# The gated stage's spatial mix as seven half-size products (one level of Strassen) in place of eight

## The chip, the cores and the metric

One Trainium2 chip, one core of it. The time is device microseconds of one execution; the number compared is the median over runs. A profiled execution gives the trace.

## The reference, cut to what matters

```python
# stage 1: a recurrence over 768 positions of 4 batches x 8 heads, state 40 x 40 (a chunked form in the kernel)
x = attention(r, k, v, w, a, b)                    # (4, 768, 320)
# stage 2: the gated block
h = np.maximum(x @ w_in, 0.0)                      # (4, 768, 1024)
u, v = h[..., :512], h[..., 512:]
v_n = (v - mean(v)) / np.sqrt(var(v) + 1e-06)      # over the 512 features of a row
v_s = np.einsum('ts,bsd->btd', w_spatial, v_n) + b_spatial[None, :, None]   # the spatial mix, 768 x 768
y = (u * v_s) @ w_out                              # (4, 768, 320)
# stage 3: a router picks one of 8 experts for each row (a row may keep its predecessor's expert),
# out = p[e] * (np.maximum(y @ w1[e], 0) @ w2[e])
```

All of it is float32.

## The kernel before, in words

The kernel is one program in which each engine has its own hand-written order of work, with semaphores between them. Stage 1 goes through 24 chunks of 32 positions and ends near 352 us. Stage 2 follows batch by batch, stage 3 tile by tile (31 tiles of 128 rows sorted by expert).

For one batch of stage 2 TensorE first makes `values` (v, six tiles of 128 tokens, 512 columns, relu'd by ScalarE into `self.v`), then the output rows `outs` of the batch before, then `gates` (u, transposed: features on partitions, 384 tokens per block, relu'd by ScalarE into `self.g`), then the spatial mix. In between VectorE has the norm of v (`norm`, in place) and, for the batch before, `routing.choose`.

The mix (`mix`, L226) works on transposed blocks: `self.v[:, s, d*128:...]` is the stationary operand, `self.wspT[:, s, t*384:...]` the moving one, s runs over the six tiles of tokens, and block j = (d, t) has d = j % 4 (128 features) and t = j // 4 (half of the 768 tokens). It fills one of two PSUM banks (D) in turns; `wait_ge(self.vs_out, n - 1)` holds a block until the gate has read the bank's last content. For each block VectorE's `gate` adds the bias out of PSUM (L293) and multiplies the gate's block in `self.g` by the sum (L297), which raises `gated`. `outs` needs all four blocks of its half of the tokens.

The routing of the batch before is spread over the mix. TensorE turns rows for it after gates j = 4 (`turn_rows`), turns the chosen experts back after mix j = 2 (`turn_back`), and counts after mix j = 3 (`count`). VectorE has, in its one queue, gate 0, `scan`, gates 1 and 2, `weigh`, gates 3 and 4, `place` (and in the last batch `first_tiles`, the table of the first eleven expert tiles), and gates 5 to 7. `scan` runs over 768 positions on one partition; SyncE's `split_rows` and `join_rows` carry its input and its result by small DMAs, and TensorE's `turn_back` waits for the latter. `weigh` waits for the turned experts, `count` for `weigh`'s one-hot rows, `place` for the counts. GpSimd scatters the batch's rows once `place` is through; SyncE fetches the first expert tiles when the scatters have landed and `first_tiles` is through.

After the last batch's mix TensorE goes on with its six output groups (L238), with the first two x tiles of stage 3 turned behind groups 3 and 4, and then with the first expert tile. `woutT` and `wgl` lie in `w1_own` during stage 1; TensorE multiplies them (`fold`) at its end and ScalarE copies the result (L157, raising `fold_d`).

Of the kernel before, what the change touches and what calls it, by code (L numbers as in the profile page):

```python
# [8 lines left out]
F32 = mybir.dt.float32  # L9
I32 = mybir.dt.int32  # L10
U32 = mybir.dt.uint32
ALU = mybir.AluOpType
# [3 lines left out]
P = 128  # L16
# [8 lines left out]
E_FF = 1024  # L25
# [21 lines left out]
GROUPS2 = TILES + 2 * ND  # L47
REST = KCH[-1][1]
# [25 lines left out]
class Gated:  # L74
# [4 lines left out]
    def __init__(self, nc, ctx, room, rows, banks, x_rows, w_in, w_spatial, b_spatial, w_out, w_gate, w_local):  # L79
# [6 lines left out]
        self.v, self.vs, self.bsp = low("v", TILES, D_HALF), low("vs", 2, TH), low("bsp", SEQ)  # L86
# [5 lines left out]
        self.wout, self.g, self.rows = sb("wout", ND, ROW), sb("g", ND, SEQ), rows  # L92
        self.stats, self.mv = sb("stats", TILES, 6), sb("mv", TILES, 2)
        self.sd, self.rs, self.half_sd, self.var = (sb(n, TILES) for n in ("sd", "rs", "half_sd", "var"))
        A, B, D, G, E = banks
        self.pair_banks = {"GE": (G[:, :], E.rearrange("p a i t -> p (a i t)")), "B": (B[:, 0], B[:, 1]),
                           "D": (D[:, 0], D[:, 1])}
        self.vs_bank, self.o_bank = (D[:, 0], D[:, 1]), (B[:, 0], B[:, 1])
# [6 lines left out]
        self.stat, self.rooted, self.normed, self.gated = sem("stat"), sem("rooted"), sem("normed"), sem("gated")  # L105
# [110 lines left out]

    def mix(self, pe, b, j):
        d, t, n = j % ND, j // ND, 2 * ND * b + j
# [4 lines left out]
        if n >= 2:  # L223
            pe.wait_ge(self.vs_out, n - 1)
        for s in range(TILES):
            mm = pe.matmul(self.vs_bank[n % 2][:, 0:TH], self.v[:, s, d * P:(d + 1) * P],  # L226
                           self.wspT[:, s, t * TH:(t + 1) * TH], start=(s == 0), stop=(s == TILES - 1))
        mm.then_inc(self.vs_made, 1)

    def outs(self, pe, b, i):  # L230
        n = TILES * b + i
        pe.wait_ge(self.gated, 2 * ND * b + ND * (1 + i * P // TH))
# [55 lines left out]
    def gate(self, dve, b, j):  # L288
        d, t, n = j % ND, j // ND, 2 * ND * b + j
        cols = slice(t * TH, (t + 1) * TH)  # L290
        dve.wait_ge(self.biased, 16)
        dve.wait_ge(self.vs_made, n + 1)
        dve.tensor_tensor(self.vs[:, n % 2, :], self.vs_bank[n % 2][:, 0:TH], self.bsp[:, cols],  # L293
                          ALU.add).then_inc(self.vs_out, 1)
        dve.wait_ge(self.vs_out, n + 1)
        dve.wait_ge(self.h_out, self.u_at(b, j) + 1)
        dve.tensor_tensor(self.g[:, d, cols], self.g[:, d, cols], self.vs[:, n % 2, :],  # L297
                          ALU.mult).then_inc(self.gated, 1)
# [376 lines left out]
def all_stages(nc, room, banks, inputs, x_rows, gated, side, routing, experts_w, experts):  # L675
# [3 lines left out]
    with ExitStack() as ctx:  # L679
# [83 lines left out]
        with nc.Block() as block:  # L763
# [79 lines left out]
            def _(pool):  # L843
# [78 lines left out]
                routing.constants(pool)  # L922
# [778 lines left out]
```

## Time and profile before

| | |
|---|---|
| median of 3 runs | 962.45 us (962.36 to 962.65) |
| the profiled execution, its own time | 962.87 us |
| its span, first to last instruction | 961.20 us |
| mean granted TensorE clock | 0.988 |
| busy: TensorE, VectorE, ScalarE, GpSimd | 935.0, 434.2, 250.9, 243.9 us |

A span is the time between the first and the last instruction. PE is TensorE (matmuls), PEld its weight loads, DVE VectorE, ACT ScalarE, POOL GpSimd, SP SyncE; a q behind an engine's name is its queue of DMAs. L226 is line 226 of the kernel. A float32 matmul stands as two records. In brackets behind a row of a timeline stands the idle time ahead of it and what ended it.

### The profile page before, as it was taken

How to read it: one execution, taken by the hardware profiler on the slowest of the kernel's cores; microseconds unless marked ns; L12 is line 12 of the kernel's file. 1: busy time of each engine (PE TensorE's matmuls, PEld its weight loads, DVE VectorE, ACT ScalarE, POOL GpSimd, SP SyncE). 2: the span in 40 equal slices, each digit the busy share in tenths (PEclk: the TensorE clock that was granted, in tenths of full speed). 3: DMA queues.
4: the chain of work that ended last, by engine and by line, in shares of the span. 5: the costliest groups of instructions: out<-in, count | busy, mean ns of one | idle time of the engine just before them, and what ended most of it. 6: DMA issues, size and time to landing. Idle time of an engine off the chain costs nothing.

```text
span 961.2 us, 54005 instructions
## 1 busy us (share of the span) xinstructions
PE 935.0 (97%) x24701; PEld 722.6 (75%) x24702; DVE 434.2 (45%) x958; ACT 250.9 (26%) x527; POOL 243.9 (25%) x226
## 2 busy tenths in 40 slices
PE   6999999999999999999999999999999999999995
PEld 6888999999999984545545555558878888888884
DVE  5476777777777633332333333253343222222220
ACT  0234444444444432002102102102122121212120
POOL 6444555445545410000020020020251011111101
PEclk8999999999999999999999999999999999999998
DMA  4265554544443325910110110329131110101000
GB/s 114 78 201 153 153 158 117 156 137 129 124 129 117 101 53 151 324 50 1 50 41 1 49 42 1 100 88 320 49 104 36 35 40 29 30 22 41 23 28 3
DMA packets 61396, 86.00 MB, mean 89 GB/s; under 512 B 22706, under 2 KB 40958, under 8 KB 61344
## 3 DMA queue, kind: packets, MB, share of 16 engines
q1 hardware_dynamic: 37232, 63.30, 21.6%
q10 hardware_dynamic: 21088, 13.32, 5.2%
q0 software_dynamic: 3024, 8.72, 2.5%
q8 instruction: 28, 0.46, 0.2%
q14 instruction: 24, 0.20, 0.1%
HBM read 72.47 MB, written 14.45 MB: 90 GB/s over the span
## 4 chain that ended last, share of the span: by engine, by line
PE 96%; issue 2%; DVE 1%; POOL 0%; ACT 0%; DVEq 0%; POOLq 0%; ACTq 0%
PE ps_D L1495 14%; PE ps_D L226 12%; PE ps_G L1477 6%; PE ps_E L1477 6%; PE ps_B L238 6%; PE ps_E L983 5%; PE ps_B L190 3%; PE ps_G L1484 3%; PE ps_D L1018 3%; PE ps_D L955 3%; PE ps_E L981 3%; PE ps_G L190 3%; PE ps_E L190 2%; PE ps_D L1056 2%; PE ps_B L960 2%; PE ps_A L960 2%
## 5 line engine op out<-in xcount | busy, mean ns | idle before, releaser
L1495 PE MATMUL ps_D<-room,hT 128*128 x496 | 139.1, 433 | 0.8 <-issue 0.8
L226 PE MATMUL ps_D<-room 128*128 128x384 f32 x384 | 126.7, 489 | 0.7 <-DVE room L293 0.7
L1495 PEld LDWEIGHTS ps_D<-room,hT 128*128 128x128 f32 x496 | 91.8, 190 | 35.9 <-issue 1.3
L226 PEld LDWEIGHTS ps_D<-room 128*128 128x128 f32 x384 | 72.1, 190 | 51.5 <-issue 1.6
L1438 POOL DMA_INDIRECT out<-y,token x31 | 35.6, 1147 | 258.3 <-DVE y L1602 225.0
L552 POOL DMA_INDIRECT sorted_rows<-rows,slot x24 | 23.9, 997 | 280.4 <-DVE slot L544 274.3
L1538 ACT ACTIVATE hT<-ps_G 128x512 f32<-128x512 f32 x31 | 18.6, 599 | 217.3 <-PE ps_E L1484 211.1
L1602 DVE TENSOR_SCALAR y<-ps_D,x_in 128x320 f32<-128x320 f32 x31 | 17.0, 550 | 126.6 <-PE ps_D L1495 118.1
L1585 DVE COPY w_own<-room 128x1024 f32 x62 | 44.8, 727 | 62.8 <-PE ps_G L1477 32.7
L293 DVE TENSOR_TENSOR room<-ps_D,room 128x384 f32<-128x384 f32 x32 | 17.8, 558 | 113.2 <-PE ps_D L226 108.2
L1237 DVE STREAM_TRANSPOSE room<-room 128x256 f32<-128x256 f32 x96 | 42.3, 441 | 53.5 <-ACT room L1125 53.5
L1477 PEld LDWEIGHTS ps_G<-xTt,w_own 128*128 128x128 f32 x496 | 59.9, 192 | 6.5 <-issue 2.3
L1477 PE MATMUL ps_G<-xTt,w_own 128*128 128x128 f32 x496 | 60.7, 276 | 1.5 <-issue 0.9
L1477 PE MATMUL ps_E<-xTt,w_own 128*128 128x128 f32 x496 | 60.5, 275 | 0.0
L1477 PEld LDWEIGHTS ps_E<-xTt,w_own 128*128 128x128 f32 x496 | 57.9, 192 | 0.0
L238 PE MATMUL ps_B<-room 128*128 128x329 f32 x192 | 54.6, 441 | 0.0
L909 POOL TENSOR_TENSOR room<-room 128x640 f32<-128x640 f32 x23 | 46.4, 2019 | 29.6 <-DVE room L1285 29.6
L885 POOL TENSOR_TENSOR room<-room 128x1024 f32<-128x1024 f32 x24 | 52.2, 2174 | 1.9
L1125 ACT ACTIVATE room<-ps_E 128x256 f32<-128x256 f32 (+1 forms) x96 | 35.0, 365 | 66.0 <-PE ps_E L983 37.3
L238 PEld LDWEIGHTS ps_B<-room 128*128 128x128 f32 x192 | 36.0, 190 | 18.4 <-issue 2.3
L983 PE MATMUL ps_E<-room 32*32 32x48 f32 (+1 forms) x3200 | 48.5, 207 | 0.8 <-issue 0.8
L1125 ACT ACTIVATE room<-room 128x512 f32<-128x512 f32 (+2 forms) x72 | 40.3, 560 | 34.5 <-PE ps_B L1034 31.1
(224 smaller groups left out, 1599.3 us busy)
## 6 DMA issues: line engine op xcount, KB each, us to landing
room<-in_moe_w SPq DMA_DIRECT2D x8, 1280.0 KB, 13.3
room<-in_moe_w SPq DMA_DIRECT2D x8, 1024.0 KB, 10.1
room<-in_vt SPq DMA_DIRECT2D x24, 320.0 KB, 3.2
room<-in_kb SPq DMA_DIRECT2D x46, 160.0 KB
x_in<-sorted_rows ACTq DMA_DIRECT2D x27, 161.0 KB, 2.2
room<-in_vo SPq DMA_DIRECT2D x24, 160.0 KB, 3.0
room<-in_rg SPq DMA_DIRECT2D x48, 80.0 KB
room<-in_r SPq DMA_DIRECT2D x48, 80.0 KB
```

What stands on the lines that cost most here:

```text
L190: pe.matmul(self.bank_of(n + g)[:, 0:width], left(g, k, slice(0, P)), right(g, k, slice(0, P)), start=(k == 0), stop=False, skip_group_che ...
L226: mm = pe.matmul(self.vs_bank[n % 2][:, 0:TH], self.v[:, s, d * P:(d + 1) * P], self.wspT[:, s, t * TH:(t + 1) * TH], start=(s == 0), stop ...
L238: mm = pe.matmul(self.o_bank[n % 2][:, 0:ROW], self.g[:, d, i * P:(i + 1) * P], self.wout[:, d, :], start=(d == 0), stop=(d == ND - 1))
L885: pool.tensor_tensor(kb_end.rearrange("p m n k t -> p (m n) k t"), raw_kb[:, :, :, :], later[:, :, None, :].broadcast_to([P, GROUPS, 2, CH ...
L909: pool.tensor_tensor(faded.rearrange("p m n e -> p (m n) e")[:, :, 0:HD], stateT.rearrange("p m n e -> p (m n) e"), whole[:, x % 4, :, Non ...
L960: mm = pe.transpose(bank[0:kept, m // 4, m % 4 * P:m % 4 * P + LIVE], src(m), ident[0:LIVE, 0:LIVE])
L983: mm = pe.matmul(E[q, :, i, kept], pw[q, i, :], powers[q, l - 2:ROUNDS - 1:ROUNDS - l, i, kept], start=True, stop=True)
L1125: act.activation(out, in_, ACT.Copy).then_inc(done, 1)
L1237: dve.transpose(pw.rearrange("p i t -> p (i t)"), (powers[:, l - 1] if l else qi[:, 0]).rearrange("p i t -> p (i t)")).then_inc(flip_d[l], 1)
L1477: mm = pe.matmul(self.ps_h[half][:, f, :], side.w1_own[:, k, col:col + P], x[:, k, :], start=(f == 0 and k == 0), stop=False, skip_group_c ...
L1495: mm = pe.matmul(self.ps_y, side.hT[:, u % 2, f, :], self.weights.w2[:, bass.ds(e, 1), f, :], start=(f == 0), stop=(f == self.NF - 1))
L1585: dve.tensor_copy(side.w1_own[:, :, cols], w1.w1[:, bass.ds(e, 1), :, cols].rearrange("p o k f -> p (o k) f")).then_inc(self.w1_in, 1)
```

## The change

The mix is a product of the 512 x 768 matrix v (transposed) and the 768 x 768 matrix of weights. Both are cut in quarters (`parts`): w into halves of the tokens summed over and of the tokens produced, v into halves of tokens and of features. Strassen's seven products of quarters replace the eight. Each product has three token tiles in place of six to sum over; each is made in two pieces c of 128 features, so a batch has 14 (`PRODUCTS`) of them, each with three matmuls of 128x128 by 384.

- Weights: five sums of quarters on GpSimd, once, four behind its constants (`sum_weights`), one when the fold is copied (`sum_last_weights`), since it lies in `w1_own`.
- Values: five sums of quarters on VectorE in each batch behind the norm (`sum_values`), ahead of `choose`.
- `gate`: each product is added to or subtracted from up to two partial sums of 384 columns in SBUF (`lower_left`, `upper_right`, `first`, `second`); four of seven products in each piece complete a block, which `times` multiplies into `self.g`. `gated` becomes a pair of semaphores, one for each half of the tokens.
- A third PSUM bank, A[:, 1], joins the two of D. TensorE's wait for `fold_d` moves ahead of the first mix; in the last batch the wait for all banks moves to the output group 3.
- The routing's steps move: `scan` behind gate 1, `weigh` behind gate 5, `place` and `first_tiles` behind gate 10; `turn_back` behind product 4, `count` behind product 8.
- New buffers lie in `hT`, in `w1_own` and in a new tensor `sums`; the scratch for software DMA is cut to 4096 bytes a partition.

```diff
+ST = TILES // 2
+PRODUCTS = 14
...
+        self.w_parts, self.v_parts = self.parts(self.wspT, TH), self.parts(self.v, D_HALF // 2)
+        sb = Carver(side.hT.rearrange("p a f n -> p (a f n)"), 0, 2 * E_FF)
+        w_top, more = sb("w_top", ST, TH), sb("more", 2, TH)
+        self.upper_right, self.lower_left, self.first, self.second = vs[:, 0], vs[:, 1], more[:, 0], more[:, 1]
+        sb = Carver(ctx.enter_context(nc.sbuf_tensor("sums", [P, ST * (TH + D_HALF)], F32)), 0, ST * (TH + D_HALF))
+        w_bottom, v_late, v_early = sb("w_bottom", ST, TH), sb("v_late", ST, D_HALF // 2), sb("v_early", ST, D_HALF // 2)
+        sb = Carver(side.w1_own.rearrange("p k f -> p (k f)"), 0, (NK - 1) * E_FF)
+        w_both, v_both = sb("w_both", ST, TH), sb("v_both", ST, D_HALF // 2)
+        self.w_sums, self.v_sums = (w_top, w_bottom, w_both), (v_early, v_late, v_both)
...
-        self.vs_bank, self.o_bank = (D[:, 0], D[:, 1]), (B[:, 0], B[:, 1])
+        self.vs_bank, self.o_bank = (D[:, 0], D[:, 1], A[:, 1]), (B[:, 0], B[:, 1])
...
+    def parts(self, x, width):
+
+        return [[x[:, i * ST:(i + 1) * ST, j * width:(j + 1) * width] for j in range(2)] for i in range(2)]
...
+    def sum_weights(self, pool):
+        (w11, w12), (w21, w22) = self.w_parts
+        top, bottom, both = self.w_sums
+        pool.wait_ge(self.loaded, 16 * self.transfers)
+        pool.tensor_tensor(top, w11, w12, ALU.add).then_inc(self.w_summed, 1)
+        pool.tensor_tensor(bottom, w21, w22, ALU.add).then_inc(self.w_summed, 1)
+        pool.wait_ge(self.w_summed, 2)
+        pool.tensor_tensor(w21, w21, w11, ALU.subtract).then_inc(self.w_summed, 1)
+        pool.tensor_tensor(w12, w12, w22, ALU.subtract).then_inc(self.w_summed, 1)
+
+    def sum_last_weights(self, pool, fold_d):
+        (w11, w12), (w21, w22) = self.w_parts
+        pool.wait_ge(fold_d, 1)
+        pool.tensor_tensor(self.w_sums[2], w11, w22, ALU.add).then_inc(self.w_summed, 1)
+
+    def sum_values(self, dve, b):
+
+        (v11, v21), (v12, v22) = self.v_parts
+        early, late, both = self.v_sums
+        dve.wait_ge(self.normed, TILES * (b + 1))
+        for k, (out, x, y, op) in enumerate(((early, v11, v12, ALU.add), (late, v21, v22, ALU.add),
+                                             (both, v11, v22, ALU.add), (v12, v12, v22, ALU.subtract),
+                                             (v21, v21, v11, ALU.subtract))):
+            if k == 3:
+                dve.wait_ge(self.v_summed, 5 * b + 3)
+            dve.tensor_tensor(out, x, y, op).then_inc(self.v_summed, 1)
+
+    def product(self, j):
+
+        (v11, v21), (v12, v22) = self.v_parts
+        (w11, w12), (w21, w22) = self.w_parts
+        (w_top, w_bottom, w_both), (v_early, v_late, v_both) = self.w_sums, self.v_sums
+        return ((v22, w21, 4, 0), (v11, w12, 4, 0), (v_early, w22, 4, 1), (v_late, w11, 4, 2), (v_both, w_both, 5, 3),
+                (v12, w_bottom, 5, 4), (v21, w_top, 5, 5))[j % 7]
+
     def mix(self, pe, b, j):
-        d, t, n = j % ND, j // ND, 2 * ND * b + j
+        n, c = PRODUCTS * b + j, j // 7
+        left, right, weights, values = self.product(j)
         if j == 0:
             pe.wait_ge(self.normed, TILES * (b + 1))
             if b == 0:
                 pe.wait_ge(self.h_out, self.u_at(0, ND) + 2)
-        if n >= 2:
-            pe.wait_ge(self.vs_out, n - 1)
-        for s in range(TILES):
-            mm = pe.matmul(self.vs_bank[n % 2][:, 0:TH], self.v[:, s, d * P:(d + 1) * P],
-                           self.wspT[:, s, t * TH:(t + 1) * TH], start=(s == 0), stop=(s == TILES - 1))
+        if b == 0 and c == 0:
+            pe.wait_ge(self.w_summed, weights)
+        if values and c == 0:
+            pe.wait_ge(self.v_summed, 5 * b + values)
+        if n >= 3:
+            pe.wait_ge(self.vs_out, n - 2)
+        for s in range(ST):
+            mm = pe.matmul(self.vs_bank[n % 3][:, 0:TH], left[:, s, c * P:(c + 1) * P], right[:, s, :],
+                           start=(s == 0), stop=(s == ST - 1))
         mm.then_inc(self.vs_made, 1)
...
     def outs(self, pe, b, i):
-        pe.wait_ge(self.gated, 2 * ND * b + ND * (1 + i * P // TH))
+        pe.wait_ge(self.gated[i * P // TH], ND * (b + 1))
...
     def gate(self, dve, b, j):
-        d, t, n = j % ND, j // ND, 2 * ND * b + j
-        cols = slice(t * TH, (t + 1) * TH)
-        dve.wait_ge(self.biased, 16)
+
+        n, c, which = PRODUCTS * b + j, j // 7, j % 7
+        made = self.vs_bank[n % 3][:, 0:TH]
+        ur, ll, one, two = self.upper_right, self.lower_left, self.first, self.second
+        if n == 0:
+            dve.wait_ge(self.biased, 16)
         dve.wait_ge(self.vs_made, n + 1)
-        dve.tensor_tensor(self.vs[:, n % 2, :], self.vs_bank[n % 2][:, 0:TH], self.bsp[:, cols],
-                          ALU.add).then_inc(self.vs_out, 1)
+        if n >= 1:
+            dve.wait_ge(self.vs_out, n)
+
+        def plus(out, x, op=ALU.add):
+            return dve.tensor_tensor(out, x, made, op)
+
+        if which == 0:
+            plus(ll, self.bsp[:, 0:TH]).then_inc(self.vs_out, 1)
+        elif which == 1:
+            plus(ur, self.bsp[:, TH:]).then_inc(self.vs_out, 1)
+        elif which == 2:
+            plus(two, ur)
+            plus(one, ll, ALU.subtract).then_inc(self.vs_out, 1)
+            self.times(dve, b, n, c, 1, two)
+        elif which == 3:
+            plus(ll, ll)
+            plus(ur, ur, ALU.subtract).then_inc(self.vs_out, 1)
+            self.times(dve, b, n, 2 + c, 0, ll)
+        elif which == 4:
+            plus(one, one)
+            plus(ur, ur).then_inc(self.vs_out, 1)
+        elif which == 5:
+            plus(one, one).then_inc(self.vs_out, 1)
+            self.times(dve, b, n, c, 0, one)
+        else:
+            plus(ur, ur).then_inc(self.vs_out, 1)
+            self.times(dve, b, n, 2 + c, 1, ur)
+
+    def times(self, dve, b, n, d, t, factor):
+        g = self.g[:, d, t * TH:(t + 1) * TH]
         dve.wait_ge(self.vs_out, n + 1)
-        dve.wait_ge(self.h_out, self.u_at(b, j) + 1)
-        dve.tensor_tensor(self.g[:, d, cols], self.g[:, d, cols], self.vs[:, n % 2, :],
-                          ALU.mult).then_inc(self.gated, 1)
+        dve.wait_ge(self.h_out, self.u_at(b, d + ND * t) + 1)
+        dve.tensor_tensor(g, g, factor, ALU.mult).then_inc(self.gated[t], 1)
...
                 routing.constants(pool)
+                gated.sum_weights(pool)
+                gated.sum_last_weights(pool, fold_d)
...
                 gated.gates(pe, 0, ND + 2)
-                for j in range(2 * ND):
+                pe.wait_ge(fold_d, 1)
+                for j in range(PRODUCTS):
                     gated.mix(pe, 0, j)
-                pe.wait_ge(fold_d, 1)
                 for b in range(1, BATCH):
                     for i in range(0, TILES, 2):
                         gated.values(pe, b, i)
...
                         gated.gates(pe, b, j)
                         if j == 4:
                             routing.turn_rows(pe, b - 1)
-                    for j in range(2 * ND):
+                    for j in range(PRODUCTS):
                         gated.mix(pe, b, j)
-                        if j == 2:
+                        if j == 4:
                             routing.turn_back(pe, b - 1)
-                        if j == 3:
+                        if j == 8:
                             routing.count(pe, b - 1)
                 experts.tensor(pe)
 
...
                 routing.convert(dve)
                 for b in range(BATCH):
                     gated.norm(dve, b)
+                    gated.sum_values(dve, b)
                     if b >= 1:
                         routing.choose(dve, b - 1)
-                    for j in range(2 * ND):
+                    for j in range(PRODUCTS):
                         gated.gate(dve, b, j)
                         if b >= 1:
-                            if j == 0:
+                            if j == 1:
                                 routing.scan(dve, b - 1)
-                            if j == 2:
+                            if j == 5:
                                 routing.weigh(dve, b - 1)
-                            if j == 4:
+                            if j == 10:
                                 routing.place(dve, b - 1)
                                 if b == BATCH - 1:
                                     routing.first_tiles(dve)
...
-        sp.wait_ge(gated.gated, 2 * ND * BATCH)
+        for done in gated.gated:
+            sp.wait_ge(done, ND * BATCH)
...
         for i in range(TILES):
             gated.outs(pe, self.LAST, i)
+            if i == 3:
+                pe.wait_ge(gated.vs_out, PRODUCTS * BATCH)
             if i >= 3 and i < 5:
                 self.turn_x(pe, 0, i - 3)
         pe.wait_ge(gated.h_out, GROUPS2 * BATCH)
-        pe.wait_ge(gated.vs_out, 2 * ND * BATCH)
...
-    nc = bacc.Bacc("TRN2", target_bir_lowering=False, num_devices=1)
+    nc = bacc.Bacc("TRN2", target_bir_lowering=False, num_devices=1, dynamic_dma_scratch_size=4096)
```

## Rows read from the trace of the kernel before

**Rows 1.** The page's busy time by engine: us, share of the span, instructions.

```profile
PE 935.0 (97%) x24701; PEld 722.6 (75%) x24702; DVE 434.2 (45%) x958; ACT 250.9 (26%) x527; POOL 243.9 (25%) x226
```

**Rows 2.** The page's chain that ended last, shares by engine.

```profile
PE 96%; issue 2%; DVE 1%; POOL 0%; ACT 0%; DVEq 0%; POOLq 0%; ACTq 0%
```

**Rows 3.** The page's groups, the mix: busy us, mean ns | idle before, releaser.

```profile
L226 PE MATMUL ps_D<-room 128*128 128x384 f32 x384 | 126.7, 489 | 0.7 <-DVE room L293 0.7
```

**Rows 4.** Timeline of VectorE in batch 0: start us, us, instruction [idle before].

```profile
404.19 0.56 DVE L293 TENSOR_TENSOR room<-ps_D,room 128x384 f32<-128x384 f32 x1 [2.72 <-PE ps_D L226]
```

**Rows 5.** Timeline of TensorE where batches 0 and 1 begin and end their mix.

```profile
388.33 4.14 PE L226 MATMUL ps_D<-room 128*128 128x384 f32 x12
...
419.40 1.88 PE L190 MATMUL ps_G<-room 128*128 128x512 f32 x4
...
461.19 11.88 PE L226 MATMUL ps_D<-room 128*128 128x384 f32 x36
...
493.05 1.88 PE L190 MATMUL ps_G<-room 128*128 128x512 f32 x4
```

**Rows 6.** Timeline of TensorE in batch 3: the mix, then the output groups.

```profile
608.49 11.88 PE L226 MATMUL ps_D<-room 128*128 128x384 f32 x36
...
641.28 9.04 PE L238 MATMUL ps_B<-room 128*128 128x329 f32 x32
```

**Rows 7.** Timeline of GpSimd's last constant and of ScalarE's copy of the fold.

```profile
343.74 0.29 POOL L417 TENSOR_SCALAR_AFFINE_SELECT upper<-upper 128x128 f32<-128x128 f32 x1
...
370.26 0.21 ACT L157 ACTIVATE room<-ps_A 128x36 f32<-128x36 f32 x1
```

**Rows 8.** GpSimd's sums at L909: duration ns min/median/max.

```profile
L909 POOL TENSOR_TENSOR room<-room x23: 1262/2091/2093, 46.5 to 341.2; 128x640 f32<-128x640 f32 x23
```

**Rows 9.** Timeline of VectorE: end of batch 0's norm, and batch 1's first routing step.

```profile
385.10 2.83 DVE L285 TENSOR_SCALAR room<-room 128x512 f32<-128x512 f32 x6
...
447.47 0.20 DVE L447 TENSOR_REDUCE top<-rows 128x6 f32<-128x48 f32 x1 [4.89 <-ACT rows L259]
```

**Rows 10.** Timeline of VectorE in batch 3: gate 0, scan, place to first_tiles, gate 5.

```profile
612.73 0.56 DVE L293 TENSOR_TENSOR room<-ps_D,room 128x384 f32<-128x384 f32 x1 [16.11 <-PE ps_D L226]
613.33 0.56 DVE L297 TENSOR_TENSOR room<-room 128x384 f32<-128x384 f32 x1
613.80 1.74 DVE L482 TENSOR_TENSOR_SCAN wide<-wide 1x768 f32<-1x768 f32 x1
...
630.08 0.25 DVE L534 TENSOR_TENSOR_SCAN upto<-inner,counts 128x48 f32<-128x48 f32 x1
...
636.70 0.56 DVE L293 TENSOR_TENSOR room<-ps_D,room 128x384 f32<-128x384 f32 x1
```

**Rows 11.** Timeline of SyncE's queue: join_rows in batch 1, the first fetches.

```profile
468.27 0.74 SPq L488 DMA_DIRECT2D turned<-wide  x1
...
642.73 3.71 SPq L1416 DMA_DIRECT2D x_in<-sorted_rows  x4
```

**Rows 12.** Busy time in one stretch; the last two columns are DMA share and GB/s.

```profile
469.60:469.90 0.30, 0.30 (x2) 0.19 (x1) 0.27 (x2) 0.00 (x0) 0.00 (x0) 1.00 0.05 10
```

**Rows 13.** DMA issues, 641 to 646 us: KB each, median us to landing.

```profile
x_in<-sorted_rows SPq DMA_DIRECT2D x3, 161.0 KB, 3.2
```

**Rows 14.** Timeline in stage 3: split_rows of the last batch and the scan behind it.

```profile
661.45 1.56 ACTq L476 DMA_DIRECT2D wide<-turned  x2
...
667.88 1.75 DVE L482 TENSOR_TENSOR_SCAN wide<-wide 1x768 f32<-1x768 f32 x1 [7.21 <-DMA wide<-turned]
```

**Rows 15.** Timeline of TensorE in stage 1, two rows behind an idle stretch.

```profile
10.72 0.35 PE L1005 MATMUL ps_A<-room 64*40 64x40 f32 x3 [2.78 <-issue]
...
73.37 0.81 PE L1028 MATMUL ps_B<-room 64*40 64x32 f32 x64 [2.90 <-issue]
```

**Rows 16.** Busy time in two stretches; third column from the end is the granted clock.

```profile
10.72:16.72 6.00, 6.00 (x181) 5.50 (x183) 2.20 (x2) 0.00 (x0) 4.64 (x6) 0.50 0.12 34
...
74.80:77.80 3.00, 3.00 (x63) 2.67 (x64) 2.05 (x3) 0.98 (x1) 2.20 (x2) 0.50 0.71 203
```

More of the change, by code:

```diff
@@ L77, with __init__ @@
     EPS = 1e-6
-    def __init__(self, nc, ctx, room, rows, banks, x_rows, w_in, w_spatial, b_spatial, w_out, w_gate, w_local):
+    def __init__(self, nc, ctx, room, side, banks, x_rows, w_in, w_spatial, b_spatial, w_out, w_gate, w_local):
         def sem(name):
@@ L85, in __init__ @@
         low = Carver(room, EARLY * EXPERT_FLOATS, FIRST_END)
-        self.v, self.vs, self.bsp = low("v", TILES, D_HALF), low("vs", 2, TH), low("bsp", SEQ)
+        self.v, vs, self.bsp = low("v", TILES, D_HALF), low("vs", 2, TH), low("bsp", SEQ)
         sb = Carver(room, FIRST_END, (EXPERTS - 1) * EXPERT_FLOATS)
@@ L91, in __init__ @@
         sb = Carver(room, (EXPERTS - 1) * EXPERT_FLOATS, ROOM)
-        self.wout, self.g, self.rows = sb("wout", ND, ROW), sb("g", ND, SEQ), rows
+        self.wout, self.g, self.rows = sb("wout", ND, ROW), sb("g", ND, SEQ), side.rows
         self.stats, self.mv = sb("stats", TILES, 6), sb("mv", TILES, 2)
         self.sd, self.rs, self.half_sd, self.var = (sb(n, TILES) for n in ("sd", "rs", "half_sd", "var"))
+        self.w_parts, self.v_parts = self.parts(self.wspT, TH), self.parts(self.v, D_HALF // 2)
[7 more added lines that the diff above has]
+        self.w_sums, self.v_sums = (w_top, w_bottom, w_both), (v_early, v_late, v_both)
         A, B, D, G, E = banks
@@ L104, in __init__ @@
         self.o_made, self.o_out = sem("o_made"), sem("o_out")
-        self.stat, self.rooted, self.normed, self.gated = sem("stat"), sem("rooted"), sem("normed"), sem("gated")
+        self.stat, self.rooted, self.normed = sem("stat"), sem("rooted"), sem("normed")
+        self.w_summed, self.v_summed, self.gated = sem("w_summed"), sem("v_summed"), (sem("gated0"), sem("gated1"))
+    def parts(self, x, width):
+        return [[x[:, i * ST:(i + 1) * ST, j * width:(j + 1) * width] for j in range(2)] for i in range(2)]
     def load(self, eng, part):
@@ L1635, in program @@
                   ctx.enter_context(nc.psum_tensor("ps_E", [P, 2, 8, CH], F32))]
-        gated = Gated(nc, ctx, room, side.rows, banks, x_rows, moe_w_in, moe_w_spatial, moe_b_spatial,
+        gated = Gated(nc, ctx, room, side, banks, x_rows, moe_w_in, moe_w_spatial, moe_b_spatial,
                       (moe_w_out, moe_w_outT), moe2_w_gate, moe2_w_local)
```

## The prediction

> **What bounds the kernel now.** I read the page's engine line first [rows 1]: TensorE is busy for 97% of the span, no other engine for half of it. The chain of waits agrees [rows 2]: 96% of what ended last is TensorE. Then the costliest groups [rows 3]: the mix keeps TensorE busy for 126.7 us and makes it wait for VectorE once, 0.7 us; VectorE's gate waits 2.72 us for TensorE ahead of each block in the undisturbed stretch [rows 4]. So time taken from the mix comes off the kernel one for one, as long as VectorE, which makes the factors, stays ahead. The question is where it falls behind.
>
> The timelines give the stage. A block of 128x384 is 12 recorded matmuls (six, two records each). From the first record to the next line's first the stage lasts 419.40 - 388.33 = 31.07 us in batch 0, 493.05 - 461.19 = 31.86 us in batch 1, whose rows batch 2 repeats [rows 5], and 641.28 - 608.49 = 32.79 us in batch 3 [rows 6]. A block takes 3.87 us: VectorE's idle of 2.72, its first instruction to the second's start (0.59) and the second's 0.56 [rows 4, 10]. Eight blocks are 30.96, 0.11 is left in batch 0. Batches 1 and 2 have 0.79 us more, TensorE's turn and count for the routing; batch 3 has 0.93 more than these, its wait for VectorE.
>
> **What is removed.** Eight blocks of 12 records become fourteen products of 6 of the same shape, 3.87/2 = 1.935 us each, 27.09 together. Each batch's stage loses 3.87 us, four lose 15.48. The group borders rise from 8 to 14; the 0.11 us left over in batch 0 bounds what eight cost, so six more cost 0 to 0.08 us. I take 0.
>
> **Weight sums on GpSimd.** Four sums of 3 x 384 = 1152 columns when its constants end at 344.03, a fifth once ScalarE has copied the fold at 370.47 [rows 7]. The nearest row is its 128x640 sum: 1.26 us at best, 2.09 in the median [rows 8], so 1152 columns cost 2.3 to 3.8 us. Four end between 353 and 359, the fifth at 374.3 at the latest, 14 us before the mix: cost 0. What they do to VectorE while the last chunk ends is bounded by 0 and the 0.83 us between those two durations; I take 0. The Trainium skill's GPSIMD Engine Reference (Specifications) speaks against such a split: GpSimd shares its SBUF interfaces with VectorE and contends with its instructions that have two SBUF inputs. By that rule the sum would be up to 0.8 us later; the spread in the row fits it and does not show the cause.
>
> **Value sums on VectorE.** Five of 768 columns after the norm. The row of 384 is 0.56 us [rows 4], so 768 cost between 0.56 and 1.12; as 384 columns more can't cost a second start, I take 0.95, 4.75 us a batch (2.8 to 5.6). The Trainium skill's page "VectorE: DVE Perf Modes" (the section on SBUF-src operations) gives a float32 tensor_tensor of N columns (N+151)/0.96 ns, 0.957 us here; by it the five are 4.8 us.
> From batch 1 on VectorE stood idle for 4.89 us after the norm, until the output rows were copied at 447.47 [rows 9]; the sums fill just that, 14 us before the mix at 461.19. Cost 0; if they take 5.6, routing's choose begins 0.7 later and TensorE turns its result 10 us later still. In batch 0 the norm ends at 387.93 [rows 9], so the sums run until 392.7 beside the mix. Products 0 and 1 need none; product 2 wants the first at 388.33 + 3.87 = 392.2, which is there at 388.9. But gate 0 queues behind all five: its bank is read out at 393.3, and product 3, the first to reuse a bank, wants that at 394.1. Cover 0.8 us, just gone at 5.6 for the five. Cost 0.
>
> **The gate's work.** Per batch it was 16 instructions of 384 columns, now 28 (20 that read a bank, 8 products). One that waits for its forerunner starts 0.59 us behind it (0.60 in the first pair), one that doesn't 0.47 to 0.48 [rows 10]. The heaviest (which = 2 and 3) take 0.48 + 0.59 + 0.48 = 1.55 us against TensorE's 1.935, and three banks leave two products of slack. In itself the gate keeps up.
>
> **The routing between gates.** The scan stood behind gate 0, whose block was seen by VectorE 612.73 - 608.49 = 4.24 us after the start (3.87 + 0.37). It now stands behind gate 1, whose product ends at the same 3.87: it starts at 4.72, lasts 1.74, ends at 6.46. SyncE's small transfer carries it back, and TensorE turns it behind product 4, at 9.68, where it was behind block 2, at 11.6. The transfer was issued at 468.27 and its bytes had moved by 469.90 [rows 11, 12]; with 0.4 for its semaphore I take 2.0, so 8.5, 1.2 us early. Gate 2, behind the scan, has read its bank by 7.6; product 5 wants it at 9.68. Weigh, eight short instructions of 0.24 us (below), is behind gate 5, whose product is seen at 12.3; gate 6 is out at 15.9, wanted at 18. Cost 0 for each.
>
> Place and first_tiles are the long block: 28 short instructions from 630.08 to 636.70, 6.62 us [rows 10]. They stood behind gate 4 of 8, with blocks 5 and 6 (7.74 us) for TensorE to work on; they now stand behind gate 10 of 14. Place alone ends batches 1 and 2, and there TensorE goes on to the next batch's values: free. In batch 3 it is not. Product 10 ends 11 x 1.935 + 0.79 = 22.08 after the start; gate 10 begins at 22.45 and its three instructions let place begin at 24.0. The block ends at 30.6. Queued behind it are gates 11 (0.48 + 0.59) and 12 (0.59 + 0.56), and the first output group waits for gate 12's factor: 32.85, on TensorE 32.9. TensorE has run out of products at 27.09 + 0.11 + 0.79 = 28.0. It stands idle for 4.9 us, and batch 3's stage is 32.9 us where it was 32.8: all of this batch's saving is given back and 0.1 more. Gate 13 ends 1.2 us later, its output group comes 6.8 us later: free.
>
> What hangs on place (scatter, then the fetch of x tiles) moves from 21.6 to 24.0 after the start, 2.4 later. The fetch went out at 642.73 [rows 11], 34.2 from the start, now 36.6; with 3.2 us to land [rows 13] it is there at 39.8. TensorE turns the first tile behind four output groups, 32.9 + 9.0 = 41.9 [rows 6]. Cover 2.1 us, cost 0. The scratch for software DMA is cut as well; no row shows what it does. What it could slow is GpSimd, busy for 25% of the span [rows 1]; I take 0, and a scatter later than the 2.1 us of cover would be paid.
>
> **The clock.** Near a TensorE that stood still the granted clock fell to 0.50, the 1.2 GHz level: from 10.72, after 2.78 us of idling, it was 0.50 for 6.0 us of work; after 2.90 us of idling up to 73.37 it was 0.50 from 74.80 to 77.80 [rows 15, 16]. The idle of 4.9 us is longer than both. Work at 1.2 GHz takes twice as long, so 3 to 6 us of it cost 1.5 to 3.0; I take 2.3. If the clock does not fall it is 0.
>
> **Sum.** 3 x 3.87 = 11.6 saved in batches 0 to 2, less 0.1 in batch 3, less 2.3 of clock: 9.2. The profiled execution takes 962.87 us (span 961.20 and 1.67 around it), so 953.7 after. The median of the runs is 0.42 lower: 953.3.
>
> **Rivals.**
> - *The stall without the clock.* TensorE waits 4.9 us but stays at 2.4 GHz. For: its 0.7 us wait in batch 3 changed nothing. Against: both waits near 3 us lowered it. 962.45 - 11.5 = 951.0.
> - *The way back is late.* The margin between scan and turn falls from 5.1 to 3.2 us, three times. For: in the last batch ScalarE had issued two such transfers by 663.01 and VectorE got them at 667.88, 4.9 us [rows 14]. Against: expert weights were loading then. At 4.9 us each turn comes 1.7 late, up to 5.1 in all: 954 to 958.4.
> - *Full saving.* VectorE's block fits after all: 962.45 - 15.5 = 947.0. It would have to begin 4.9 us earlier; nothing speaks for it.
> - *VectorE becomes the bound (slower).* Per batch 28 gate instructions and 5.5 us of scan, weigh and place stand in a stage that was 31.1 us. It decides from (31.1 - 5.5)/28 = 0.91 us each; at 1.12 (twice 0.56) a batch takes 36.9 us, 5.8 x 4 = 23 more: 985. Against: the rows of 384 columns, with an input in PSUM or both in SBUF, are all 0.56.
> - *No change.* Half-length groups cost 0.65 us more each at their six new borders. Against: 0.11 left for eight.
>
> **How the numbers follow.** My forecast 0.60 (own range 952.3 to 954.9); stall without clock 0.14; way back late 0.15; full saving 0.03; slower 0.05; no change 0.03. The range 950.5 to 957.5 takes in the first two and most of the third. 0.2% (1.9 us) is about what a measurement of this kernel can tell from no change. Faster 0.92, same 0.03, slower 0.05.
>
> **What would show it.** The mix's group at 126.7 x 7/8 = 111 us and 336 records; stages of 27.2 us in batch 0, 28.0 in 1 and 2; in batch 3 one idle of about 4.9 us before the first output group, released by VectorE's gate; the granted clock at 0.50 for some us behind it. I am wrong if TensorE waits between the products or at the turn in batches 1 and 2, if the short VectorE block is not what the output group waits for, or if the clock stays up.

## The result, and the profile after

| | before | changed |
|---|---|---|
| median | 962.44 us (962.36 to 962.65, 4 runs) | 950.57 us (949.40 to 952.38, 4 runs) |
| profiled execution, span | 962.87, 961.20 us | 952.38, 950.6 us |
| ratio | | 0.9876, 95% interval 0.9864 to 0.9889 |

The kernel is 11.9 us faster; 953.3 was forecast, with 950.5 to 957.5 as the range. The median lies at the range's very edge, outside my own narrower range of 952.3 to 954.9, and nearer to the 951.0 of the rival "the stall without the clock" than to my figure. The time alone would have picked that rival; the trace rules it out, since the clock did fall. Stage 2 came out as forecast, wait and low clock included; 1.2 to 3.3 us more came from an edit that I had priced at nothing, the cut of the DMA scratch.

The timeline of TensorE shows batch 0 from its first product to its last and the line behind it, then the ends of batch 1; these answer to [rows 5].

```profile
391.11 4.14 PE L282 MATMUL ps_D<-room 128*128 128x384 f32 x12
395.08 2.10 PE L282 MATMUL ps_A<-room,sums 128*128 128x384 f32 x6
397.02 2.10 PE L282 MATMUL ps_D<-room,sums 128*128 128x384 f32 x6
...
416.37 2.10 PE L282 MATMUL ps_D<-hT,room 128*128 128x384 f32 x6
418.30 1.88 PE L206 MATMUL ps_G<-room 128*128 128x512 f32 x4
...
460.09 2.20 PE L282 MATMUL ps_A<-room 128*128 128x384 f32 x6
...
488.08 1.88 PE L206 MATMUL ps_G<-room 128*128 128x512 f32 x4
```

Products start 1.93 to 1.94 us apart behind the first (2.04), in three banks in turns, without an idle mark. Batch 0 lasts 418.30 - 391.11 = 27.19 us, batch 1 27.99 (forecast 27.2 and 28.0); batch 2, from 529.87 to 557.86, 27.99 too.

Batch 3 answers to [rows 6]. Same view, TensorE:

```profile
599.65 4.14 PE L282 MATMUL ps_D<-room 128*128 128x384 f32 x12
...
625.71 2.10 PE L282 MATMUL ps_D<-hT,room 128*128 128x384 f32 x6
632.46 11.57 PE L294 MATMUL ps_B<-room 128*128 128x329 f32 x32 [4.66 <-DVE room L384]
643.87 0.49 PE L1553 MATMUL ps_A<-ident,x_in 128*128 128x128 f32 x3
```

And VectorE there (L620 opens place, L684 first_tiles, L356 and L384 are the gate's sum and product); it answers to [rows 10]:

```profile
623.57 0.25 DVE L620 TENSOR_TENSOR_SCAN upto<-inner,counts 128x48 f32<-128x48 f32 x1
...
625.41 0.07 DVE L684 MEMSET first<- 128x9 f32 x1
...
630.06 0.17 DVE L678 CAST tile_expert<-wide 128x11 int32<-128x11 f32 x1
630.14 0.55 DVE L356 TENSOR_TENSOR hT<-hT,ps_A 128x384 f32<-128x384 f32 x1
630.61 0.55 DVE L356 TENSOR_TENSOR room<-room,ps_A 128x384 f32<-128x384 f32 x1
631.26 0.55 DVE L356 TENSOR_TENSOR hT<-hT,ps_D 128x384 f32<-128x384 f32 x1
631.85 0.56 DVE L384 TENSOR_TENSOR room<-room,hT 128x384 f32<-128x384 f32 x1
```

Place begins 23.92 us behind the stage's start (forecast 24.0), the four gate instructions stand in a row behind first_tiles, and the last of them ends at 632.41, 0.05 ahead of the output groups. The stage lasts 32.81 us; before it was 32.79. The wait is where and as long as forecast. Behind it the 32 records of four output groups take 11.57 us where they took 9.04 [rows 6]. The busy times with the granted clock (third column from the end) say why:

```profile
632.46:636.80 4.34, 4.34 (x8) 2.85 (x9) 2.60 (x5) 0.00 (x0) 0.96 (x1) 0.50 0.20 76
640.00:645.00 5.00, 5.00 (x21) 3.49 (x20) 0.00 (x0) 1.44 (x5) 0.00 (x0) 1.00 0.94 303
```

TensorE works at 1.2 GHz at first (0.50), at 2.4 GHz again later (1.00).

The spans differ by 961.2 - 950.6 = 10.6 us. By sections: the start of the first mix comes 2.78 us later (391.11 against 388.33); from there to the output groups of batch 3 it is 11.60 us less (241.35 against 252.95); from there to the first expert tile's second product 2.53 more (clock); the tiles 1.2 less (all but 0.1 of it at tile 5, which e6 and e11 come back to); behind the last tile's second product (939.89, before 947.39) 3.1 less. The first of these can't be put down to the change: over the 13 profiles of this study, most of them with the same stage 1, the first mix starts between 387.4 and 391.1 us (both ends are kernels with the change, the two without it start at 388.3 and 389.4), and the stretches at 1.2 GHz in the first 90 us differ from one execution to the next.

The last of them is a term that the forecast did not have. GpSimd's last DMA, before, changed, and in the experiment e1:

```profile
953.43 0.98 POOL L1438 DMA_INDIRECT out<-y,token  x1 [4.40 <-DVE y L1602]
```

```profile
945.93 0.98 POOL L1528 DMA_INDIRECT out<-y,token  x1 [4.39 <-DVE y L1693]
```

```profile
955.33 0.98 POOL L1438 DMA_INDIRECT out<-y,token  x1 [4.39 <-DVE y L1602]
```

The span ends 7.8 us behind its issue before (961.2), 4.7 in the changed kernel (950.6) and 4.7 in e1 (960.0).

### The profile page after: what moved, and what is told of

It reads as the page before. It is cut to its first block, busy times and chain, and to the rows that moved or that the text cites. A ratio compares the mean times of both kernels' runs of the same rounds, so it can differ in the third digit from the quotient of the medians.

```text
span 950.6 us, 54027 instructions
## 1 busy us (share of the span) xinstructions
PE 924.5 (97%) x24653; PEld 717.5 (75%) x24654; DVE 475.2 (50%) x1026; ACT 249.8 (26%) x527; POOL 255.6 (27%) x231
## 4 chain that ended last, share of the span: by engine, by line
PE 97%; issue 2%; DVE 1%; POOL 0%; ACT 0%; DVEq 0%; POOLq 0%; ACTq 0%
PE ps_D L1585 14%; PE ps_D L282 7%; PE ps_B L294 6%; PE ps_G L1567 6%; PE ps_E L1567 6%; PE ps_E L1071 5%; PE ps_A L282 4%; PE ps_B L206 3%; PE ps_G L1574 3%; PE ps_D L1043 3%; PE ps_D L1106 3%; PE ps_E L1069 3%; PE ps_G L206 3%; PE ps_E L206 2%; PE ps_D L1144 2%; PE ps_B L1048 2%
## 5 line engine op out<-in xcount | busy, mean ns | idle before, releaser
L294 PE MATMUL ps_B<-room 128*128 128x329 f32 x192 | 57.1, 456 | 4.7 <-DVE room L384 4.7
L1006 POOL TENSOR_TENSOR room<-room 128x256 f32<-128x256 f32 x24 | 15.6, 649 | 127.5 <-DVE room L1417 127.5
L1071 PEld LDWEIGHTS ps_E<-room 32*32 32x32 f32 x3200 | 41.2, 105 | 6.9 <-issue 5.9
L1213 ACT ACTIVATE room<-ps_D 128x1024 f32<-128x1024 f32 x24 | 24.6, 1025 | 49.6 <-PE ps_D L1043 49.6
```

Source lines behind the costliest of these rows:

```text
L294: mm = pe.matmul(self.o_bank[n % 2][:, 0:ROW], self.g[:, d, i * P:(i + 1) * P], self.wout[:, d, :], start=(d == 0), stop=(d == ND - 1))
L1071: mm = pe.matmul(E[q, :, i, kept], pw[q, i, :], powers[q, l - 2:ROUNDS - 1:ROUNDS - l, i, kept], start=True, stop=True)
L1213: act.activation(out, in_, ACT.Copy).then_inc(done, 1)
```

## The experiments

**e1: the scratch alone.** The kernel before with

```diff
-    nc = bacc.Bacc("TRN2", target_bir_lowering=False, num_devices=1)
+    nc = bacc.Bacc("TRN2", target_bir_lowering=False, num_devices=1, dynamic_dma_scratch_size=4096)
```

> The kernel before with nothing but the scratch for software DMA cut to 4096 bytes. Theory (the gain is the mix's alone): within 0.1% of 962.4 us, and the span ends 7.8 us after GpSimd's last DMA is issued, as before. Rival (the cut of the scratch gives part of the gain): about 959.3 us, 3.1 us less, all of it behind that last issue, where the changed kernel needs 4.7 us instead of 7.8.

Measured: 961.15 us against 963.36 on this chip, 0.9977 (0.9966 to 0.9988): 1.2 to 3.3 us. The rival holds. In the trace it is the 3.1 us at the end shown above; the mixes stay as they were.

**e2: work in TensorE's wait.**

```diff
         gated, routing = self.gated, self.routing
+        pe.wait_ge(gated.h_out, GROUPS2 * BATCH)
+        for _ in range(10):
+            pe.matmul(gated.pair_banks["GE"][0][:, 0:256], gated.wout[:, 0, 0:P], gated.wout[:, 0, 0:256],
+                      start=True, stop=True)
         for i in range(TILES):
             gated.outs(pe, self.LAST, i)
```

> The changed kernel with ten idle-time matmuls of 256 columns (20 records of 0.21 us, 4.3 us; their result is not used) put between the last batch's product 13 and the first output group, where TensorE waits 4.7 us for VectorE. Theory (the wait lowers the clock, and the low clock costs 2.5 us of the output groups): the first 32 records of the output groups take about 9.0 us in place of 11.57, their start stays where it was, and the kernel is 2.5 us faster than the changed one, about 948.0 us. Rival (the clock is not what makes them slow, or it falls for another reason): 950.5 us, and 11.6 us for the 32 records.

Measured: 0.9864 (0.9849 to 0.9878) of before, so 1.2 us less than the changed kernel's 0.9877 (e5), inside the intervals. TensorE's timeline and the clock of the stretch:

```profile
624.93 4.48 PE L1600 MATMUL ps_G<-room 128*128 128x256 f32 x20
629.75 9.15 PE L294 MATMUL ps_B<-room 128*128 128x329 f32 x32 [0.34 <-issue]
```

```profile
629.75:638.70 8.95, 8.95 (x32) 6.12 (x33) 2.59 (x5) 1.33 (x3) 0.95 (x1) 1.00 0.45 117
```

The start of the output groups stays where it was (32.8 us behind 596.94), the clock stays up, and the 32 records take 9.15 us in place of 11.57: the theory holds for the place. The forecast of 948.0 us does not: the kernel keeps only part of the gain. From the first tile's second product to the last it now takes 2.1 us longer than in the changed kernel (654.7 to 940.9 against 659.9 to 944.0), in tiles 5 and 6 (see e6 and e11).

**e3: first_tiles behind the gates.**

```diff
                             if j == 10:
                                 routing.place(dve, b - 1)
-                                if b == BATCH - 1:
-                                    routing.first_tiles(dve)
+                            if j == 13 and b == BATCH - 1:
+                                routing.first_tiles(dve)
```

> The changed kernel with first_tiles moved in the last batch from behind gate 10 to behind gate 13; place stays. Theory (the 4.8 us of first_tiles queued ahead of gates 11 and 12 are the wait of TensorE): the output groups begin 28.0 us after the start of the mix in place of 32.8, without a wait. But the fetch of the first x tiles waits for the scatters of place and for first_tiles, 36.6 us after the start, lands at 39.8, and TensorE wants the first tile at 37.0: a new wait of 2.8 us there, with or without a fall of the clock. 950.6 - 7.4 + 2.8 = 946 us, 948.5 if the clock falls. Rival (something else holds the output groups, as the expert loads or ScalarE): 950 us or slower.

Measured: 0.9866 (0.9851 to 0.988), 950.46 us: hardly a gain. TensorE, ScalarE and GpSimd:

```profile
624.07 4.71 PE L294 MATMUL ps_B<-room 128*128 128x329 f32 x16
632.44 6.36 PE L294 MATMUL ps_B<-room 128*128 128x329 f32 x16 [3.66 <-ACT rows L315]
```

```profile
631.85 0.78 ACT L315 ACTIVATE rows<-ps_B 128x329 f32<-128x329 f32 x2 [17.13 <-DMA sorted_rows<-rows,slot]
```

```profile
629.02 0.96 POOL L638 DMA_INDIRECT sorted_rows<-rows,slot  x1 [0.30 <-issue]
```

The theory was right on the first point: the output groups begin 28.05 us behind the start (596.02) without a wait. What comes next is not the fetch, as I had written (946 to 948.5 us); it is what the rival named, ScalarE, and the time is the rival's too: ScalarE's copy of the output rows is late. It writes into `rows`, which the scatters of the batch before still read, so it waits until GpSimd's sixth scatter (issued at 629.02) has landed; after two groups both banks are full, and TensorE waits 3.7 us and then works at 1.2 GHz again for 3.4 us. From the first product of batch 3's mix to the first tile's second product (654.64) that leaves 58.6 us in place of 60.2, and tiles 5 and 6 of stage 3 take 1.9 back. The scatters start with place, so place itself has to come earlier.

**e4: place earlier, first_tiles later.**

```diff
-                        if j == 8:
+                        if j == 7:
                             routing.count(pe, b - 1)
...
-                            if j == 10:
+                            if j == 8:
                                 routing.place(dve, b - 1)
-                                if b == BATCH - 1:
-                                    routing.first_tiles(dve)
+                            if j == 12 and b == BATCH - 1:
+                                routing.first_tiles(dve)
```

> The changed kernel with TensorE's count behind product 7 (was 8), place behind gate 8 (was 10) in all batches, and in the last batch first_tiles behind gate 12 (was behind place). Theory: gates 11 and 12 come at their products, the output groups begin 28.0 us after the mix's start, the scatters are sent 4.8 us earlier, and the first x tile is there before TensorE wants it. No wait, no low clock: 950.6 - 4.8 - 2.5 = 943.3 us. Rival (the gates behind the earlier place fall behind and TensorE waits for a bank, or the fetch is late): a wait between products or at the first x tile, 945 to 948 us.

Measured: 945.21 us against 963.36, 0.9804 (0.9789 to 0.9819); run again as e10:

> The earlier place with the later first_tiles once more, beside the next one on the same chip: 0.9804 of the kernel before, tiles 4 to 6 of stage 3 10.1 and 10.6 us apart in its trace.

943.39 against 964.68, 0.9787 (0.9774 to 0.98). That is 0.007 to 0.009 less than the changed kernel's 0.9877, 7 to 8.6 us; 7.3 were forecast. In e4's trace the mix starts at 597.97 and the output groups follow without a wait and at full clock:

```profile
624.03 2.10 PE L282 MATMUL ps_D<-hT,room 128*128 128x384 f32 x6
625.96 9.04 PE L294 MATMUL ps_B<-room 128*128 128x329 f32 x32
```

27.99 us, and 9.04 for the 32 records. That is the forecast's 4.8 and 2.5 us, 7.3 together, in the place where they were to come. The rival's 945 to 948 us take in the first median, but no wait of its kind, between products or at the first x tile, is in the trace. From the mix's first product of batch 0 to the end, though, e4's trace is only 5.2 us shorter than the changed kernel's (943.7 - 389.43 against 950.6 - 391.11), as tiles 4 to 6 take 2.1 us longer; e10's is 6.7 shorter. No version of the study has a clearly lower ratio.

**e5: the changed kernel again.**

> The changed kernel once more, as it is, to stand beside the others on one chip. 0.9876 of the kernel before, within 0.15%. In its trace stage 1 may end up to 3 us earlier or later (the clock in its first 90 us), the mixes of batches 0 to 2 last 27.2, 28.0 and 28.0 us, and the wait in batch 3 is 4.7 us.

Measured: 950.98 us (949.57 to 952.57) against 962.25, 0.9877 (0.9862 to 0.9892), as expected, and the wait is 4.67 us. Behind it the 32 records take 12.17 us, so here the low clock costs 3.1 us where it cost 2.5 in the first profile.

**e6 and e11: VectorE's second table in two pieces**, on top of e4. The calls; `other_tiles` itself is divided where its table begins:

```diff
-        routing.other_tiles(dve)
-        self.peeled(dve, self.tile_dve, 4, FIRST - 2)
+        routing.other_tiles(dve, 0)
+        self.peeled(dve, self.tile_dve, 4, 5)
+        routing.other_tiles(dve, 1)
+        self.peeled(dve, self.tile_dve, 5, FIRST - 2)
```

> The kernel with the earlier place and the later first_tiles, and besides VectorE's second table (other_tiles, 6 us behind tile 3 of stage 3) cut in two, its second part behind tile 4. Theory: VectorE's 6 us in one piece make its copies of the expert weights late for two tiles of stage 3, where TensorE waited 0.4 and 0.9 us and the tiles stood 10.1 and 10.6 us apart in place of 9.45; in two pieces of 2.6 and 3.5 us they are hidden: 1.8 us less than with the earlier place alone, 9 to 10 us less than the changed kernel, ratio to it 0.990. Rival (those waits are the fetch of x tiles or the scatters): the tiles stay 10.1 and 10.6 apart, 0.992 of the changed kernel.

Measured: 943.12 us, 0.9804 (0.979 to 0.9817) of before, as e4, and 0.992 of the changed kernel on the same chip (950.98), which is the rival's figure and not the theory's 0.990. In its trace all tiles up to the last two are 9.45 to 9.9 us apart, as the theory has it. So again, beside e10:

> The same with VectorE's second table in two pieces. Theory: 1.8 us (0.19%) less than the one before it in this list, with all tiles 9.45 to 9.9 us apart. Rival (the tiles were late by chance, and the pieces bring nothing): no difference in the times.

Measured: 946.60 against e10's 943.39 on one chip, 3.2 us slower. Its tiles 5 and 6 are 12.3 us apart. TensorE at tile 5:

```profile
699.24 1.61 PE L1591 MATMUL ps_D<-room,hT 128*128 x5
701.08 0.70 PE L1591 MATMUL ps_D<-room,hT 128*128 x2 [0.23 <-issue]
702.53 1.15 PE L1591 MATMUL ps_D<-room,hT 128*128 x3 [0.74 <-issue]
703.96 1.88 PE L1591 MATMUL ps_D<-room,hT 128*128 x6 [0.28 <-issue]
```

It stops in the middle of a group of 16, where it waits for no engine that the profile shows. The theory falls: e10, which has the block of 6 us in one piece, had one gap of 10.0 us, e4 two, of 10.1 and 10.6, and e11, with the block in two pieces, one of 12.3.

The 13 traces show something that comes ahead of the block. VectorE's copy of the last expert weights in tile 3, in e4 and in the changed kernel:

```profile
681.48 0.43 DVE L1680 COPY w_rest_own<-room 128x512 f32 x1 [2.04 <-remote]
```

```profile
688.85 0.65 DVE L1680 COPY w_rest_own<-room 128x512 f32 x1 [0.41 <-PE ps_E L1574]
```

In the changed kernel it follows TensorE's matmul after 0.41 us. In e4 it comes some 1.6 us later, released by a signal that the profile can't match with an instruction ("remote"), and ScalarE's next step, which waits for the same signal of TensorE, starts late with it (681.43). VectorE's block of 6 us begins behind that, at 686.99. So it is in all eight traces with late tiles (before, e1, e2, e3, e4, e9, e10, e11: 1.98 to 2.08 us of idle ahead of this copy), and in none of the other five (changed, e5, e6, e7, e8: 0.41), of which four have the block in one piece and lose nothing by it. e6 and e11 are the same kernel, one on each side. So e6 was no test of the theory. What holds TensorE's signals back in tile 3, and what stops it in tile 5 of e11, is open.

**e7: two banks.**

```diff
-        if n >= 3:
-            pe.wait_ge(self.vs_out, n - 2)
+        if n >= 2:
+            pe.wait_ge(self.vs_out, n - 1)
...
-            mm = pe.matmul(self.vs_bank[n % 3][:, 0:TH], left[:, s, c * P:(c + 1) * P], right[:, s, :],
+            mm = pe.matmul(self.vs_bank[n % 2][:, 0:TH], left[:, s, c * P:(c + 1) * P], right[:, s, :],
...
-        made = self.vs_bank[n % 3][:, 0:TH]
+        made = self.vs_bank[n % 2][:, 0:TH]
```

> The changed kernel with the two banks of D in turns, without the third. Theory (the gate keeps up, slack of one product is nearly enough): TensorE waits 1.1 us in batch 0 at product 2, behind the five value sums, and 1.0 us at product 13 in batches 1 and 2, where place stands; in batch 3 product 13 waits 5.8 us, the output groups start 33.8 us after the mix's start. 4.1 us more than the changed kernel in all. Rival (the gates of two sums hold TensorE at every turn): 10 us or more.

Measured: 953.40 us, 0.9913 (0.99 to 0.9927), 3.5 us more than the changed kernel. TensorE's four waits:

```profile
393.41 4.11 PE L282 MATMUL ps_D<-room,sums 128*128 128x384 f32 x12 [0.66 <-DVE room L356]
...
485.29 2.20 PE L282 MATMUL ps_D<-hT,room 128*128 128x384 f32 x6 [0.58 <-DVE room L356]
...
555.92 2.20 PE L282 MATMUL ps_D<-hT,room 128*128 128x384 f32 x6 [0.58 <-DVE room L356]
...
631.31 4.21 PE L282 MATMUL ps_D<-hT,room 128*128 128x384 f32 x6 [5.34 <-DVE room L356]
```

At product 2 of batch 0 and product 13 of the others, as forecast; batches 0 to 2 last 0.84 to 0.90 us longer than in the changed kernel (1.0 to 1.1 forecast), some 0.25 more than the idle mark counts, as the last record outlasts its start-to-start time. In batch 3 the output groups start 35.6 us after the mix's start, not 33.8: product 13 itself now runs at 1.2 GHz (six of its records in 4.21 us, elsewhere 2.10), and the 32 records behind it take 9.47 in place of 11.57. The gates themselves hold nobody.

**e8: more value sums in batch 0.**

```diff
+        self.extra = sem("extra_sums")
...
         dve.wait_ge(self.normed, TILES * (b + 1))
+        if b == 0:
+            for out, x, y in ((early, v11, v12), (late, v21, v22), (both, v11, v22)):
+                dve.tensor_tensor(out, x, y, ALU.add).then_inc(self.extra, 1)
+            dve.wait_ge(self.extra, 3)
```

> The changed kernel with the first three of the value sums made twice in batch 0, which puts 2.7 us more of VectorE's work ahead of gate 0. Theory (the sums are hidden in batch 0 with a cover of 0.8 to 1.0 us only): product 3 of batch 0 waits for its bank 1.7 us, the mix of batch 0 lasts 28.9 us in place of 27.2, and the kernel is 1.7 us slower than the changed one. Rival (the cover is larger, as VectorE runs ahead again): no wait, 27.2 us.

Measured: 951.91 us, 0.9897 (0.9881 to 0.9912), 1.9 us more than the changed kernel. TensorE in batch 0:

```profile
387.77 4.14 PE L287 MATMUL ps_D<-room 128*128 128x384 f32 x12
391.74 2.10 PE L287 MATMUL ps_A<-room,sums 128*128 128x384 f32 x6
395.29 2.17 PE L287 MATMUL ps_D<-room,sums 128*128 128x384 f32 x6 [1.45 <-DVE room L361]
...
416.65 1.88 PE L207 MATMUL ps_G<-room 128*128 128x512 f32 x4
```

Product 3 waits, the batch lasts 28.88 us, 1.7 more than without the extra sums. These took 2.73 us (387.40 to 390.13), so the slack ahead of product 3 was 1.0 us, the upper end of the 0.8 to 1.0 worked out.

**e9: the turn behind product 2.**

```diff
-                        if j == 4:
+                        if j == 2:
                             routing.turn_back(pe, b - 1)
```

> The changed kernel with TensorE's turn of the expert row behind product 2 (was 4), so that TensorE has to wait for the way back from VectorE's scan and the wait can be read. The turn is reached 5.8 us after the mix's start. Theory (scan ends at 6.46, the small transfer takes 2.0 us): it is done at 8.5, TensorE waits 2.7 us in batches 1, 2 and 3, and the kernel is 8.1 us slower than the changed one. Rival (the way back takes 3.2 us or more and the margin in the changed kernel is nothing): 3.9 us a batch or more, 11.7 us slower.

Measured: 959.48 us, 0.9946 (0.9932 to 0.9961), 6.6 us more than the changed kernel. The chain by who waited for whom (line waited for: us in total, times, longest):

```profile
PE ps_A L579 <- DMA turned<-wide: 7.0, 3, 2.6
```

TensorE's first such wait, and VectorE's scan ahead of it:

```profile
465.64 0.22 PE L579 MATMUL ps_A<-ident,turned 6*128 6x6 f32 x1 [2.18 <-DMA turned<-wide]
```

```profile
462.04 1.74 DVE L568 TENSOR_TENSOR_SCAN wide<-wide 1x768 f32<-1x768 f32 x1
```

The way back takes 1.9 us in batches 1 and 2 and 2.3 us in batch 3 (609.54 to 611.81). In the changed kernel the scan of batch 1 ends 6.4 us after the mix's start and the turn stands at 9.9 (469.96), so the margin behind product 4 is 1.6 us there and 1.2 in batch 3; 1.2 was forecast for all. The trace's stages are 2.3, 4.0 and 2.7 us longer, 8.9 together against 8.1 forecast: behind the wait in batch 2 the clock fell too (0.58 from 539 to 543), which costs 1.7 us. The medians differ by less, 6.6 us.

## Why the prediction was right, point by point

GpSimd's first weight sum and one of VectorE's value sums in the changed kernel, for the points below:

```profile
346.89 2.63 POOL L237 TENSOR_TENSOR hT<-room 128x1152 f32<-128x1152 f32 x1
```

```profile
392.48 0.95 DVE L258 TENSOR_TENSOR w_own<-room 128x768 f32<-128x768 f32 x1
```

- **Removed.** 27.19 and 27.99 us for 27.2 and 28.0. Six more borders cost nothing that the trace shows. Mix, wait and low clock together give 11.60 - 2.53 = 9.07 us, 9.2 forecast: the mechanism was right, and this is the part of the time that it explains.
- **Weight sums.** GpSimd took 2.63 us for each sum of 1152 columns (bounds 2.3 and 3.8); four ended at 357.4, the fifth at 375.9, 15 us ahead. Between ScalarE's two copies of 1024 columns around the sums it is 16.37 us (344.16 to 360.53), 16.48 in the kernel before (341.27 to 357.75), so stage 1 was not slowed. Of the rule of the Trainium skill's GPSIMD Engine Reference (Specifications) on the shared SBUF interfaces these sums show no effect: they take 2.63 us beside the last chunk and 2.62 behind it.
- **Value sums.** 390.74 to 395.30, 4.56 us (forecast 4.75). Hidden, and e8 shows how narrowly. One takes 0.95 us; the formula of the Trainium skill's page "VectorE: DVE Perf Modes" (the section on SBUF-src operations) gives 0.957, and this row agrees.
- **Gates, scan, turn, weigh.** No wait between products. e7 shows that the gates need the third bank by less than 1 us a batch (batch 3 apart), e9 the margin of the turn (1.2 to 1.6 us). The margin of weigh was not tested. One reading was off without effect: in the kernel before the scan ended 4.8 us ahead of the turn, not 5.1 (its rows in batch 3: 613.80 + 1.74, the turn at 620.30).
- **Place and first_tiles.** A wait of 4.66 us by the idle mark and 4.8 by the stage (32.81 - 27.99; forecast 4.9), and this batch's saving lost. The x tiles were fetched at 636.22, 36.6 us after the start as forecast, and nothing waited for them. e4 takes the wait away by the order alone.
- **Clock.** 11.57 - 9.04 = 2.53 us (forecast 2.3 of 1.5 to 3.0), 3.1 in e5, a little over the upper bound. e2 shows that it hangs on the idle TensorE.
- **The step that was mis-sized** is the scratch, "I take 0": it is worth 3.1 us in the trace and 1.2 to 3.3 by the times (e1). I had looked for its price at GpSimd's issues, where nothing changed, and not behind the last one. 953.3 less 2 to 3 us is 950.3 to 951.3; measured are 950.57 and 950.98. That this sum closes is in part luck: the profiles also differ by a start 2.8 us later and by tile 5, 1.1 us, and neither is in it. That the median stayed inside the range, by 0.07 us, is luck as well.
- **Of the rivals** none came. The way back is not late (e9: 1.9 to 2.3 us, where the rival had 4.9), VectorE is no bound (0.55 us for each of the gate's instructions), the clock did fall.

## What to carry to other kernels

When a stage gets shorter, the fixed blocks of small work queued in its helper engine do not: look for the longest piece between two results that the bounding engine waits for, and count how much of the stage is left behind it. Four batches had the same saving and one lost it all to 6.6 us of routing; moving two blocks, and no arithmetic, brought it back with interest, in the place itself. And moving one block alone (e3) only uncovered the next wait, so follow what hangs on the block that stays.

## What the runs showed of the hardware that I had not expected

- With 4096 bytes of DMA scratch a partition the span ends 4.7 us after the last software DMA is issued, with the default 7.8 (e1, the same kernel otherwise). What is done in these 3.1 us no row shows.
- The changed kernel's times spread over 949.4 to 952.4 us. In its profiled execution the granted clock was at 1.2 GHz for some 24 us of the first 90, in the profile of before for 13.6, with the same work in both.
- In tile 3 of stage 3 TensorE's signal reaches VectorE and ScalarE some 1.6 us late in eight of the 13 traces and in time in five, in two runs of the same kernel (e6, e11) once each; where it is late, tiles 4 to 6 take 0.5 to 2.9 us more. A gain of 2 us ahead of it (e2) can vanish there.
- TensorE can stop for 0.2 to 0.7 us in the middle of a group of matmuls without a wait on any engine that the profile shows (e11, tile 5), and that tile came 2.9 us late.
